# Attention with top-32, gated mixing and a Fourier block on one core: the exponential one slot later, eight places for small lists, first transposes ahead of the last projection

## The reference

```python
# 1. attention, 8 heads of 64: only the 32 highest scores of a row take part
scores = scale * q @ k.T                        # 576 x 576 for each batch and head
kth = np.partition(scores, -32, axis=-1)[..., -32:-31]
scores = np.where(scores >= kth, scores, -1e9)
attn = exp(scores - max); attn /= attn.sum() + 1e-9
x = attn @ v
# 2. gated mixing: causal convolution with 5 taps for each feature
gate = sigmoid(sum(conv_w[k] * x_shifted[k])); x = (gate * (x @ w_val)) @ w_out
# 3. Fourier block: 2-D FFT's real part, layer norm, two products with 2048 hidden features
u = x + real(fft(fft(x, axis=1), axis=2))
un = (u - mean) / sqrt(var + 1e-6)
out = u + relu(un @ w_ch1) @ w_ch2
```

## Time and profile before

| | |
|---|---|
| median of 3 runs | 1215.79 us (1215.04 to 1216.76) |
| the profiled execution | 1214.56 us, its span 1212.8 us |
| granted TensorE clock, mean | 0.926 of full speed |
| busy: TensorE | 1049.4 us (87%) |
| busy: VectorE | 884.3 us (73%) |
| busy: ScalarE | 621.3 us (51%) |
| busy: POOL | 406.9 us (34%) |

### The profile page before, as it was taken

One profiled execution on the slowest core, in us unless ns is written; L12 is line 12 of the kernel. 1 busy time (PEld: TensorE's weight loads), 2 busy tenths in 40 slices (PEclk: granted clock), 3 DMA queues, 4 the chain that ended last, 5 costly groups with the idle time before them and its releaser, 6 DMA issues.

```text
span 1212.8 us, 19844 instructions
## 1 busy us (share of the span) xinstructions
PE 1049.4 (87%) x6608; PEld 841.9 (69%) x6608; DVE 884.3 (73%) x1898; ACT 621.3 (51%) x1253; POOL 406.9 (34%) x704
## 2 busy tenths in 40 slices
PE   3776565789798989989798989999798999998998
PEld 2554454666587878866587878775587888648887
DVE  6999999996996978696996978696996970330000
ACT  3786766644565655554565655454565653012221
POOL 2444533142443332233433332322443322133221
PEclk9886756889898999999898999999898999998999
DMA  8566455021355856321355846321365655206974
GB/s 256 163 202 203 140 187 188 11 74 35 102 209 193 282 192 198 134 75 46 111 217 192 270 178 213 123 70 45 126 226 202 226 179 204 108 1 237 351 277 162
DMA packets 81188, 200.37 MB, mean 165 GB/s; under 512 B 8384, under 2 KB 26560, under 8 KB 81088
## 3 DMA queue, kind: packets, MB, share of 16 engines
q1 hardware_dynamic: 81088, 199.11, 48.2%
HBM read 177.58 MB, written 21.50 MB: 164 GB/s over the span
## 4 chain that ended last, share of the span: by engine, by line
PE 56%; issue 14%; DVE 12%; POOL 10%; ACT 5%; DMA 1%; SPq 1%; DVEq 0%; ACTq 0%; POOLq 0%
PE p_m L567 15%; PE p_m L553 15%; PE p_m L461 14%; DVE rest L742 5%; PE p_t L434 4%; PE p_t L450 4%; PE p_s L421 4%; DVE top L748 3%; ACT prob L630 2%; POOL k_lo L876 2%; POOL bias L884 1%; POOL hid_lo L949 1%; POOL w_st L901 1%; POOL bias L885 1%; DMA u<-w_ch 1%
## 5 line engine op out<-in xcount | busy, mean ns | idle before, releaser
L748 DVE MAX8 top<-rest 128x8 f32<-128x576 f32 x432 | 304.7, 747 | 0.0
L949 POOL TENSOR_TENSOR hid_lo<-hid,hid_hi 128x256 fp32r<-128x256 f32 (+1 forms) x128 | 107.0, 836 | 325.8 <-ACT hid_hi L692 325.8
L742 DVE MATCH_REPLACE8 rest<-top,rest 128x576 f32<-128x576 f32 x288 | 211.7, 743 | 0.0
L553 PE MATMUL p_m<-un_hi,w_st 128*128 128x320 f32 (+1 forms) x1024 | 172.9, 313 | 44.6 <-POOL un_lo L940 25.3
L567 PE MATMUL p_m<-w_st,hid_hi 128*128 128x512 f32 x640 | 206.3, 404 | 0.2 <-POOL hid_lo L949 0.2
L553 PEld LDWEIGHTS p_m<-un_hi,w_st 128*128 128x128 f32 x1024 | 149.6, 198 | 55.5 <-POOL un_lo L940 26.2
L630 ACT ACTIVATE prob<-s_sb,bias 128x576 f32<-128x576 f32 x144 | 111.1, 772 | 105.0 <-POOL bias L885 104.6
L623 ACT ACTIVATE s_sb<-p_s 128x576 f32<-128x576 f32 x144 | 93.1, 646 | 136.3 <-PE p_s L421 136.2
L434 PE MATMUL p_t<-id_sb,prob 128*128 128x128 f32 x720 | 122.1, 306 | 34.4 <-ACT or_sb L652 34.0
L421 PE MATMUL p_s<-k_hi,q_st 128*128 128x512 f32 (+1 forms) x320 | 118.2, 372 | 33.2 <-POOL k_lo L876 19.5
L450 PE MATMUL p_t<-pT,v_sb 128*64 128x128 f32 (+1 forms) x1600 | 106.9, 285 | 43.5 <-ACT pT L643 23.4
(11 more groups left out here) (78 smaller groups left out, 1602.9 us busy)
## 6 DMA issues: line engine op xcount, KB each, us to landing
w_st<-w_split SPq DMA_DIRECT2D x256, 512.0 KB, 4.4
w_split<-w_st SPq DMA_DIRECT2D x32, 512.0 KB, 3.0
q_raw<-qT SPq DMA_DIRECT2D x64, 144.0 KB, 3.4
k_raw<-kT SPq DMA_DIRECT2D x64, 144.0 KB, 3.4
u<-w_ch SPq DMA_DIRECT2D x32, 256.0 KB, 3.6
v_sb<-v SPq DMA_DIRECT2D x16, 256.0 KB, 3.5
wslot<-w_val SPq DMA_DIRECT2D x4, 1024.0 KB, 5.3
wslot<-w_out SPq DMA_DIRECT2D x4, 1024.0 KB, 5.3
```

Source lines behind the costliest of these rows:

```text
L553: mm = pe.matmul(mbank(HIDDEN_BANK[g], n), w1_st[i % NB1][:, w, k, :], x[:, k, at:at + n], start=part + k == 0, stop=part + k == KC + 1)
L742: dve.match_replace(rest[tt % 2][:, :], top[tt % 4][:, 8 * n - 8:8 * n], src[:, :], LOWEST).then_inc(s_chain, 1)
L748: found = dve.max(top[tt % 4][:, 8 * n:8 * n + 8], rest[tt % 2][:, :])
L949: pool.tensor_tensor(hid_lo[i % 2][:, 0:WIDTH[g]], hid[:, 0:WIDTH[g]], hid_hi[i % 2][:, 0:WIDTH[g]].bitcast(F32), ALU.subtract).then_inc(m ...
```

## The change

The rectifier and the exponential of tile t, with POOL's two numbers for it, stand in slot t + 5. The lists `top`, `bias`, `psum_row` and `rinv` have eight places, and the waits for an old place look eight tiles back. In the list of steps the transposes of the first normalised block stand ahead of `seq` 2, those of the second ahead of `proj` 4, and the two normalisations stand at `proj` 1 and `proj` 2. In a batch with attention beside it, `proj` 3 and `trn` 0 fall in one slot (slot 88 for the second batch), `seq` 2 and `trn` 1 in the next (89), `proj` 4 and `ch0` 0 in the third (90); before it was `proj` 3, then `seq` 2, `trn` 0 and `proj` 4, then `trn` 1 and `ch0` 0. No other step changes its slot. No instruction is added or taken away.

```diff
+NK = 8
-STEPS += [("seq", 0), ("proj", 0), ("proj", 1), ("seq", 1), ("proj", 2), ("proj", 3), ("seq", 2), ("trn", 0), ("proj", 4),
-          ("trn", 1)]
+STEPS += [("seq", 0), ("proj", 0), ("proj", 1), ("seq", 1), ("proj", 2), ("proj", 3), ("trn", 0), ("seq", 2), ("trn", 1),
+          ("proj", 4)]
-NORM_AT = {("proj", 2): 0, ("seq", 2): 1, ("ch0", 1): 2, ("ch0", 4): 3, ("ch0", 7): 4}
+NORM_AT = {("proj", 1): 0, ("proj", 2): 1, ("ch0", 1): 2, ("ch0", 4): 3, ("ch0", 7): 4}
-SELECT, EXPONENT, RECIP, TRANSPOSE, ATTEND = 1, 4, 6, 6, 7
+SELECT, EXPONENT, RECIP, TRANSPOSE, ATTEND = 1, 5, 6, 6, 7
-        top = [sb(f"top{i}", [P, TOPK]) for i in range(4)]
-        bias = [sb(f"bias{i}", [P, 2]) for i in range(4)]
+        top = [sb(f"top{i}", [P, TOPK]) for i in range(NK)]
+        bias = [sb(f"bias{i}", [P, 2]) for i in range(NK)]
-        psum_row = sb("psum_row", [P, 4])
-        rinv = sb("rinv", [P, 4])
+        psum_row = sb("psum_row", [P, NK])
+        rinv = sb("rinv", [P, NK])
                     act.activation(prob[t % 3][:, 0:S], s_sb[t % NS][:, :], ACT.Prelu,
-                                   bias=bias[t % 4][:, 1:2], scale=-BIG, alpha=1.0 / BIG).then_inc(s_drop, 1)
-                    if t >= 4:
-                        act.wait_ge(s_radd, (t - 4) // 2 + 1)
+                                   bias=bias[t % NK][:, 1:2], scale=-BIG, alpha=1.0 / BIG).then_inc(s_drop, 1)
+                    if t >= NK:
+                        act.wait_ge(s_radd, (t - NK) // 2 + 1)
...
-                            if tt >= 4:
-                                dve.wait_ge(s_bias, 2 * (tt - 3))
+                            if tt >= NK:
+                                dve.wait_ge(s_bias, 2 * (tt - NK + 1))
...
                     dve.wait_ge(s_exp, t + 1)
-                    if t >= 4:
-                        dve.wait_ge(s_pv, unit_of(t - 4) + 1)
+                    if t >= NK:
+                        dve.wait_ge(s_pv, unit_of(t - NK) + 1)
...
                     pool.wait_ge(s_topk, t + 1)
-                    if t >= 4:
-                        pool.wait_ge(s_exp, t - 3)
+                    if t >= NK:
+                        pool.wait_ge(s_exp, t - NK + 1)
```

More of the change, by code:

```diff
@@ L630, in exponent @@
                     act.activation(prob[t % 3][:, 0:S], s_sb[t % NS][:, :], ACT.Prelu,
[L631 to L633 removed]
+                                   bias=bias[t % NK][:, 1:2], scale=-BIG, alpha=1.0 / BIG).then_inc(s_drop, 1)
+                    if t >= NK:
+                        act.wait_ge(s_radd, (t - NK) // 2 + 1)
                     act.wait_ge(s_drop, t + 1)
                     act.activation(prob[t % 3][:, 0:S], prob[t % 3][:, 0:S], ACT.Exp,
[L636 to L637 removed]
+                                   bias=bias[t % NK][:, 0:1], scale=-SCALE,
+                                   accum_out=psum_row[:, t % NK:t % NK + 1]).then_inc(s_exp, 1)
                 def store_pT(t):
@@ L730, in select @@
                             dve.wait_ge(s_copy, tt + 1)
-                            if tt >= 4:
-                                dve.wait_ge(s_bias, 2 * (tt - 3))
-                            dve.max(top[tt % 4][:, 0:8], s_sb[tt % NS][:, :]).then_inc(s_chain, 1)
+                            if tt >= NK:
+                                dve.wait_ge(s_bias, 2 * (tt - NK + 1))
+                            dve.max(top[tt % NK][:, 0:8], s_sb[tt % NS][:, :]).then_inc(s_chain, 1)
                             count[0] += 1
@@ L741, in select @@
                             src = s_sb[tt % NS] if n == 1 else rest[tt % 2]
-                            dve.match_replace(rest[tt % 2][:, :], top[tt % 4][:, 8 * n - 8:8 * n], src[:, :],
+                            dve.match_replace(rest[tt % 2][:, :], top[tt % NK][:, 8 * n - 8:8 * n], src[:, :],
                                               LOWEST).then_inc(s_chain, 1)
@@ L747, in select @@
                             dve.wait_ge(s_chain, done[tt])
-                            found = dve.max(top[tt % 4][:, 8 * n:8 * n + 8], rest[tt % 2][:, :])
+                            found = dve.max(top[tt % NK][:, 8 * n:8 * n + 8], rest[tt % 2][:, :])
                             if n == TOPK // 8 - 1:
@@ L767, in reciprocal @@
                     dve.wait_ge(s_exp, t + 1)
-                    if t >= 4:
-                        dve.wait_ge(s_pv, unit_of(t - 4) + 1)
-                    c = slice((t - 1) % 4, (t - 1) % 4 + 2)
+                    if t >= NK:
+                        dve.wait_ge(s_pv, unit_of(t - NK) + 1)
+                    c = slice((t - 1) % NK, (t - 1) % NK + 2)
                     dve.tensor_scalar(rinv[:, c], psum_row[:, c], EPS_SUM, 2.0, ALU.add, ALU.mult).then_inc(s_radd, 1)
@@ L880, in biases @@
                     pool.wait_ge(s_topk, t + 1)
-                    if t >= 4:
-                        pool.wait_ge(s_exp, t - 3)
-                    most, kth = top[t % 4][:, 0:1], top[t % 4][:, TOPK - 1:TOPK]
-                    pool.tensor_scalar(bias[t % 4][:, 1:2], kth, BIG, None, ALU.mult).then_inc(s_bias, 1)
-                    pool.tensor_scalar(bias[t % 4][:, 0:1], kth, most, SCALE, ALU.subtract, ALU.mult).then_inc(s_bias, 1)
+                    if t >= NK:
+                        pool.wait_ge(s_exp, t - NK + 1)
+                    most, kth = top[t % NK][:, 0:1], top[t % NK][:, TOPK - 1:TOPK]
+                    pool.tensor_scalar(bias[t % NK][:, 1:2], kth, BIG, None, ALU.mult).then_inc(s_bias, 1)
+                    pool.tensor_scalar(bias[t % NK][:, 0:1], kth, most, SCALE, ALU.subtract, ALU.mult).then_inc(s_bias, 1)
                 def scale_out(t):
```

2 lines of the change are left out of this document (1 added, 1 removed).

## The result

The changed kernel takes 1207.13 us (median of 4 runs, 1205.41 to 1207.93) against 1215.65 us of the kernel before on the same chip (4 runs): a ratio of 0.9927, 95% interval 0.991 to 0.9944. The forecast was 1211.4 us. The profiled execution took 1205.41 us with a span of 1203.6 us, 9.2 us less than the span before.

A forecast was written before the change was run, and what follows sets the result against it. VectorE was taken to bound the first stage, TensorE the rest. First stage +4.3, batches -6.0, slot 102 +2.2 and last batch -4.9 sum to -4.4 us, giving 1211.4 us; own range 1206 to 1216, with rivals 1200 to 1222.

The forecast's parts named there:

- proof against me: Sign named beforehand: a first stage of equal length, or a middle period shorter by 4 us, would prove the prediction wrong.
- the term of the clock: First hidden chunk of each batch with attention: TensorE back at full clock, less a slower projection 4; 1.0 us net gain.
- First stage, +4.3: Slots up to 43: VectorE's reciprocals wait for the later exponential; 4.3 us lost, bounds 1.6 and 7.7.
- The wait in slot 9: First stage: VectorE's reciprocal, starting at 48.30, would wait for the exponential ending at 50.63; 2.3 us.
- The bias of slot 17: First stage: POOL's 1.57 us bias would finish before VectorE's two subtractions start, taking its usual 0.22; 1.35 us come back.
- Batches, -2.0 each: Transposes ahead of the last projection in three batches with attention: 2.0 us gained each, bounds +1 and -9.
- all three new waits: TensorE idle for the next pair's keys, the attention output's copy, and VectorE's additions of projection 4: 2.1, 2.6, 1.1 us.
- Slot 102, +0.75 each: Middle, after a slot of only 2.6 us: TensorE's transposes wait for the later exponential; 0.75 us, three times, 2.2 us lost.
- Last batch, -4.9: Batch without attention: first hidden chunk 2.6 us earlier, second chunk's slow clock gone for 2.3; bounds -6.2 and -2.0.
- No gain from the lag in the middle: Middle: ScalarE's 24.3 us of waits for POOL's biases stay despite the later exponential; no gain booked.
- B: Rival, chance 0.2: first stage loses the whole 7.7 us, batches give nothing (+0.5 each); slower, 1224.6 us.
- A: Rival, chance 0.2: VectorE pays only 1.6 us in the first stage, batches give 5 us each; 1197.5 us.

## Why the prediction was right, and where its sizes were off

The sign, the places and most of the mechanisms were right; the sum was -4.4 us on a span that fell by 9.2. The time of 1207.1 us is near the lower end of the forecast's own range (1206 to 1216). The period got 3.6 us shorter, not 1.3, which is close to the 4 us that I had named as proof against me, and the scores of slot 43 came 5.0 us later, not 4. That the gain was not smaller is in part luck, as the term of the clock shows.

**First stage, +4.3:** measured +4.95 at slot 46. The kind of cost was right, its make-up only in part. The wait in slot 9 that I put at 2.3 us was 0.15 (the reciprocal waits 0.26, 1.20 and 0.95 us in slots 13, 15 and 19 instead, and the whole is 2.6 us, where I had 5.7 by slot 19). ScalarE was 1.5 us earlier at the start here; in the run with the lag alone, which started later, slot 9 waited 1.92 us. The bias of slot 17 did slip ahead of VectorE's subtractions and took its usual 0.22 us:

```profile
95.93 0.22 POOL L885 TENSOR_SCALAR bias<-top 128x1 f32<-128x1 f32 x1
...
96.59 0.80 DVE L761 TENSOR_TENSOR q_st<-q_raw,q_st 64x512 fp32r<-64x512 f32 x2
```

What I put at nothing is that the shifted instructions also meet new neighbours. From 14 to 258 us VectorE's `gate` instructions take 14.3 us instead of 13.0 and its `rinv` ones 6.3 instead of 5.2; with the 2.6 us of waits that is 5.0 us, the size of the loss. Two examples of the kernel after:

```profile
166.08 2.56 DVE L790 SCALAR_TENSOR_TENSOR gate<-x_new,cw_sb,gate 128x576 f32<-128x576 f32 x2
166.38 1.65 POOL L902 TENSOR_TENSOR w_st<-u,w_st 128x512 fp32r<-128x512 f32 x1 [2.37 <-ACT w_st L662]
...
193.46 1.40 POOL L875 TENSOR_TENSOR q_st<-q_raw,q_st 64x576 fp32r<-64x576 f32 x1 [6.29 <-ACT k_hi L618]
193.66 1.28 DVE L772 TENSOR_SCALAR rinv<-psum_row 128x2 f32<-128x2 f32 x1
```

Two `gate` instructions take 0.82 us each when alone; here the second took 1.72. The reciprocal's first part takes 0.17 us at the median and 1.28 beside POOL's subtraction. The Trainium skill (SBUF — State Buffer, Who interferes with whom) says that of a VectorE and a GpSimd instruction that need the shared port the one issued first holds it for its whole length; these rows agree, with the one that started second as the long one each time (POOL's subtraction of 166.38 began under the first `gate` and took 1.65 us instead of 1.28, the second `gate` began under it). The rows of slot 17 before do not tell the order: POOL's bias began 0.02 us ahead of VectorE's subtraction and was still the long one.

The first stage is also less certain than one profile shows. Over the profiled executions of all kernels the scores of slot 45 start at 246.1 to 248.1 us with the lag of four (six kernels), and at 251.4 to 258.2 with five and the biases in their old place (seven kernels, mean 254.2): the lag costs some 7 us there on average (slot 4 starts at 23.0 and 22.8 us on average), with 5 in the pair of profiles above. The spread goes with the start, where ScalarE waits for the DMA of the first weights. In the kernel after:

```profile
19.10 0.63 ACT L662 ACTIVATE w_st<-u 128x512 fp32r<-128x512 f32 x1 [2.59 <-DMA u<-w_ch]
```

In the one with the waits filled from their start:

```profile
23.70 0.63 ACT L665 ACTIVATE w_st<-u 128x512 fp32r<-128x512 f32 x1 [7.16 <-DMA u<-w_ch]
```

With four slots this is caught up (slot 4 starts at 21.2 to 25.0 us, slot 45 within 2 us). With five, VectorE waits for the late exponentials: 2.6 us in all in the first of the two, 5.4 in the second.

**Batches, -2.0 each:** around the transposes the difference was -1.6 us a batch (slots 82 to 92 of the second), with all three new waits where I had put them: 1.86 for 2.1 us, 2.45 for 2.6, 0.96 for 1.1, and VectorE's 1.0 us for POOL's power. Of the clock's two sides here the loss was larger than I had it, 1.5 us on projection 4 (5.13 for 3.65) for my 0.8, and a wait of TensorE of 0.68 us in slot 94, which I had not priced, is gone (0.4 us). With it a batch gave 2.0 us: this part was right.

**What was mis-sized is the clock's term.** I priced it for the first hidden chunk alone ("I take 1.0 us as the net gain of the clock"). But TensorE's unchanged waits in slots 98 and 108 (4.70 and 3.13 us before, 4.65 and 3.12 after) also became cheaper. Slot 98 and slot 108 of the kernel before:

```profile
645.48:661.66 16.18, 11.48 (x74) 10.02 (x73) 9.73 (x19) 7.03 (x16) 7.96 (x11) 0.79 0.46 149
719.75:730.95 11.20, 8.07 (x31) 7.29 (x32) 11.09 (x23) 6.11 (x13) 4.22 (x9) 0.70 0.21 84
```

The same slots of the kernel after stand above, with a clock of 0.89 and 0.83: 0.8 and 1.2 us shorter. There are three of the one kind and two of the other, 4.8 us in all, which is as much as the gap between the forecast and the result. In the kernel before the clock fell 0.8 to 1.8 us ahead of the end of these waits, in the kernel after from 0.1 us ahead to 1.4 us behind, and the stretch at half clock was the short one. For slots 62, 98 and 134 that goes with the new order in most kernels that keep POOL's old order: 15.1 to 15.4 us in seven of them, 16.1 to 16.2 in the three with the old steps (the run with the transposes behind the exponential has the new steps and 15.8). Slots 72 and 108 are not safe: 9.98 us here, 10.85 and 8.42 with the order alone, 10.9 in both with the second normalisation at projection 3. So their 2.4 us were luck of timing as much as a gain of the change, and why the fall comes to lie where it does stays open.

**Slot 102, +0.75 each:** the wait is there, 0.4 us. **Last batch, -4.9:** -4.8 (2.75 us earlier at the first chunk, the rest from the clock behind it). **No gain from the lag in the middle:** right, by the runs with the lag alone and from tile 38 on, as long as POOL's order stays. **Eight places, nothing:** no gain; a cost of up to 2 us isn't excluded.

Of the rivals, B's first part (7.7 us in the first stage) is nearer to the mean of seven kernels than my 4.3; its second part, batches that give nothing, fell. A's wait for `un_lo` did go, but with new waits, as I had argued.

## What to carry to other kernels

When a small instruction lets the next engine go, look at what stands ahead of it in its own queue before giving it a later slot: swapping two calls on POOL was worth 27 us, a slot of slack cost 10, and still 4 with the calls swapped. Price a wait of TensorE as its length and the half-clock stretch behind it, at every place where it waits and not only at the one edited, and as a range: the same wait of 3.12 us made slots from 8.4 to 11.2 us long. And where one engine is full, a change that moves it against its neighbours needs a range from several executions: two that differed by 4.6 us in slot 4 were 6.6 us apart in slot 45, with the same instructions up to there.

## What was new about the hardware here

- The same wait of 3.12 to 3.13 us made slots of 11.20, 9.98, 8.42 and 10.85 us (slot 108 before, after and with the order alone, and slot 72 with the order alone). At 8.42 the clock did not fall at all (granted 1.00), at 10.85 it was 0.69:

```profile
448.49:459.34 10.85, 7.72 (x31) 7.05 (x32) 10.74 (x23) 6.11 (x13) 4.08 (x9) 0.69 0.22 87
714.89:723.31 8.42, 5.30 (x31) 4.72 (x31) 8.32 (x17) 6.11 (x13) 3.11 (x7) 1.00 0.28 112
```

  The order alone also had a wide spread over its five runs, 1193.0 to 1200.8 us.
- The stretch at half clock may begin behind the wait, on running work: 1.4 us after it in slot 108 of the kernel after. The Trainium skill (TensorE: Matmul & The Clock Gate, What's actually happening) says that the slow level is the default and activity releases it; the filled waits agree: with TensorE kept at work for 2.3 of 3.1 us the clock stayed at 1.00.
- A throwaway transpose of 128x128 took 0.12 us at full clock (2.29 us for 19) and 0.23 in slot 45 of the run that had them behind the exponential (3.89 us for 17). Those that lay within a wait cost nothing: slot 108 got 1.55 us shorter with them.
